# Two heads' score products in the row halves of TensorE, and first weights split ahead of the first group's rows: attention and two expert layers on one core

## The reference

```python
scores = scale * np.matmul(q, k.transpose(0, 1, 3, 2))
kth = np.partition(scores, -top_k, axis=-1)[..., -top_k:-top_k + 1]
mask = scores >= kth
scores = np.where(mask, scores, -1000000000.0)
scores = scores - np.max(scores, axis=-1, keepdims=True)
attn = np.exp(scores)
attn = attn / (np.sum(attn, axis=-1, keepdims=True) + 1e-09)
...
for e in range(E):
    mask = e_idx == e
    h = np.maximum(x[mask] @ w1[e], 0.0)
    out[mask] = gate_w[mask, None] * (h @ w2[e])
...
for e in range(E):
    h = np.maximum(x @ w1[e], 0.0)
    out += p[:, e:e + 1] * (h @ w2[e])
```

## Time and profile before

| | |
|---|---|
| median of 3 runs | 956.07 us (955.36 to 958.46) |
| the profiled execution | 953.17 us, its span 951.4 us |
| TensorE busy | 903.7 us, 95% of the span |
| VectorE busy | 557.8 us, 59% |
| ScalarE busy | 340.6 us, 36% |
| GpSimd busy | 286.1 us, 30% |
| mean granted TensorE clock | 0.957 of 2.4 GHz |

### The profile page before, as it was taken

One profiled execution on the slowest core, in us unless ns is written; L12 is line 12 of the kernel. 1 busy time (PEld: TensorE's weight loads), 2 busy tenths in 40 slices (PEclk: granted clock), 3 DMA queues, 4 the chain that ended last, 5 costly groups with the idle time before them and its releaser, 6 DMA issues.

```text
span 951.4 us, 13448 instructions
## 1 busy us (share of the span) xinstructions
PE 903.7 (95%) x4813; PEld 758.7 (80%) x4813; DVE 557.8 (59%) x1103; ACT 340.6 (36%) x726; POOL 286.1 (30%) x231
## 2 busy tenths in 40 slices
PE   5999999997999999993899799999999999999998
PEld 4888888886767667662778699989998998889897
DVE  4999999999999989752365334233223321332121
ACT  3545555553546555413364411212112220222010
POOL 7676667646775665304111020000000000000000
PEclk8589999996999999987999999999999999999999
DMA  9130000005332434325548160022002100000001
GB/s 221 48 111 23 7 18 12 12 13 198 123 111 100 163 113 147 118 95 186 191 145 288 36 243 1 1 89 89 1 1 89 54 34 0 0 0 0 33 11 55
DMA packets 49395, 75.61 MB, mean 79 GB/s; under 512 B 24624, under 2 KB 24624, under 8 KB 49328
## 3 DMA queue, kind: packets, MB, share of 16 engines
q1 hardware_dynamic: 42160, 61.09, 18.7%
q0 software_dynamic: 4160, 13.63, 4.6%
q10 hardware_dynamic: 3008, 0.05, 0.2%
HBM read 63.49 MB, written 11.27 MB: 79 GB/s over the span
## 4 chain that ended last, share of the span: by engine, by line
PE 75%; issue 10%; POOL 9%; DMA 3%; SPq 1%; DVE 1%; ACT 1%; PEld 1%; PEldq 0%; POOLq 0%; DVEq 0%; ACTq 0%
PE bank L1376 19%; PE bank L1377 18%; PE bank L1378 18%; PE bank L1432 6%; POOL att L633 6%; PE bank L1511 4%; PE bank L1371 4%; PE bank L1527 3%; POOL att L636 2%; PE bank L1403 2%; PE bank L1401 1%; DMA w_raw<-in_moe_w_dram 1%; DMA q_raw<-in_q_dram 1%; DMA xs_raw<-x_a,a_tok_i 1%; PE bank L1540 1%
## 5 line engine op out<-in xcount | busy, mean ns | idle before, releaser
L633 POOL TENSOR_SCALAR att<-sc,top 128x576 f32<-128x576 f32 x70 | 120.8, 1726 | 122.2 <-DVE top L1060 111.4
L1060 DVE MAX8 top<-work 128x8 f32<-128x576 f32 x216 | 152.0, 743 | 0.1
L1376 PE MATMUL bank<-xT,w1h 128*128 128x384 f32 x384 | 129.3, 337 | 5.3 <-DVE w1l L1255 5.3
L1313 DVE SCALAR_TENSOR_TENSOR hT<-bank,hT 128x384 fp32r<-128x384 f32 x96 | 52.9, 557 | 130.5 <-ACT hT L957 130.1
L1378 PE MATMUL bank<-xT,w1h 128*128 128x384 f32 x384 | 128.9, 336 | 0.0
L1377 PE MATMUL bank<-xT,w1l 128*128 128x384 f32 x384 | 128.9, 336 | 0.0
L957 ACT ACTIVATE hT<-bank 128x384 fp32r<-128x384 f32 x96 | 46.9, 492 | 200.5 <-PE bank L1378 200.5
L1376 PE MATMUL bank<-w2h,hT 128*128 128x512 f32 x288 | 112.2, 390 | 1.2 <-DVE hT L1313 1.2
L1432 PE MATMUL bank<-v_one,attT 128*128 128x65 f32 (+3 forms) x800 | 111.7, 281 | 0.8 <-ACT av L768 0.6
L1378 PE MATMUL bank<-w2l,hT 128*128 128x512 f32 x288 | 112.2, 390 | 0.0
L1377 PE MATMUL bank<-w2h,hT 128*128 128x512 f32 x288 | 112.2, 389 | 0.0
(11 more groups left out here) (266 smaller groups left out, 1524.0 us busy)
## 6 DMA issues: line engine op xcount, KB each, us to landing
w_raw<-in_moe_w_dram SPq DMA_DIRECT2D x96, 512.0 KB, 6.0
q_raw<-in_q_dram SPq DMA_DIRECT2D x18, 128.0 KB, 2.7
v_one<-in_v_dram POOLq DMA_DIRECT2D x18, 128.0 KB, 5.8
out_dram<-x_tok SPq DMA_DIRECT2D x9, 256.0 KB, 2.0
k_raw<-in_k_dram SPq DMA_DIRECT2D x8, 256.0 KB, 5.2
y_dram<-zero POOLq DMA_DIRECT2D x2, 1024.0 KB, 6.7
y_dram<-b_ys POOLq DMA_DIRECT2D x7, 256.0 KB, 2.8
x_dram<-x_cur SPq DMA_DIRECT2D x6, 256.0 KB, 7.1
```

Of the source, the lines that this page charges most:

```text
L633: nc.gpsimd.tensor_scalar(att[:, g % ATR, :], sc[:, g % RING, :], top8[:, g % RING, 3, 7:8], None, ALU.is_ge).then_inc(keep_made, 1)
L1060: nxt = nc.vector.max(out=top8[:, g % RING, i + 1, :], in_=work[:, j, :])
L1313: nc.vector.scalar_tensor_tensor(out=hTl(b)[:, f, :], in0=bank[:, HB + f % 4, 0:BW], scalar=0.0, in1=f32(hTh(b)[:, f, :]), op0=ALU.max, op ...
L1376: nc.tensor.matmul(dst, high_lhs, high_rhs, start=start, stop=False)
```

## The change

1. `scores(p)` makes, at an even step p, the first 288 columns of the two heads p and p + 1, and at the odd step the other 288 columns of both. The six matmuls of a step alternate between the partition halves, one head's product into bank `SB`, the other's into `SB + 1`. The count of matmuls and their shapes stay.
2. `copy_scores` writes half the columns of two buffers instead of one whole buffer; at an even step it waits until one more head is done before it overwrites. VectorE now starts both heads of a pair when the second step's copy is made.
3. In tile 4 `att_times_v` alternates between the two column halves of the array for each chunk of the contraction, instead of finishing one half first.
4. `dense_products` gives 5 instead of 4 outside tile 4, 3 instead of 2 where only the scores are of tile 4, 4 instead of 2 where only the values' product is, and 2 instead of 0 where both are.
5. Where attention ends ScalarE splits the first piece of weights, then makes the exponentials, then splits the other three, and only then copies group a's fifth result.

```diff
+        def pair_half(p):
+            return p - p % 2, slice(p % 2 * HS, (p % 2 + 1) * HS)
...
-            def copy_scores(g):
-                act.wait_ge(sc_made, g + 1)
-                if g >= RING:
-                    act.wait_ge(att_made, g - RING + 1)
-                nc.scalar.activation(sc[:, g % RING, :].rearrange("p (a b) -> p a b", a=2), bank[:, SB:SB + 2, 0:HS],
+            def copy_scores(p):
+                g, cols = pair_half(p)
+                act.wait_ge(sc_made, p + 1)
+                if p == g and g >= RING:
+                    act.wait_ge(att_made, g + 1 - RING + 1)
+                nc.scalar.activation(sc[:, g % RING:g % RING + 2, cols], bank[:, SB:SB + 2, 0:HS],
...
-            act.wait_ge(GB.lsub_made, 3)
-            nc.scalar.activation(GB.lg_b[:, :, :], GB.lg_a[:, :, :], ACT.Exp).then_inc(GB.lexp_made, 1)
             with act.If(guarded(act, GA, SPREAD)):
+                group_exponents()
+                a_copy_y(SPREAD - 1)
                 a_rare_slots()
+                split_high(0, w1_raw, w1h, w1_loaded, w1_high)
             with act.Else():
+                split_high(0, w1_raw, w1h, w1_loaded, w1_high, (0,))
+                group_exponents()
+                split_high(0, w1_raw, w1h, w1_loaded, w1_high, (1, 2, 3))
+                a_copy_y(SPREAD - 1)
                 act.drain().then_inc(a_ys, GA.slots - SPREAD)
-            split_high(0, w1_raw, w1h, w1_loaded, w1_high)
...
-                    dve.wait_ge(sc_copied, g + 1)
+                    dve.wait_ge(sc_copied, g0 + 2)
...
-                for i in range(2):
-                    cols = slice(i * HS, (i + 1) * HS)
-                    for j, (high, low, b) in enumerate(parts):
-                        last = product(bank[:, SB + i, 0:HS], high[pp, h // 2, :], low[pp, h // 2, :],
-                                       kTh[b][pp, h // 2, cols], kTl[b][pp, h // 2, cols], j == 0, j == len(parts) - 1)
+                pairs = [both for high, low, b in parts for both in ((high, kTh[b]), (low, kTh[b]), (high, kTl[b]))]
+                for j, (query, key) in enumerate(pairs):
+                    for i in range(2):
+                        pp = slice(D * i, D * i + D)
+                        last = nc.tensor.matmul(bank[:, SB + i, 0:HS], query[pp, c, :], key[pp, c, cols], start=(j == 0), stop=(j == len(pairs) - 1))
...
-                for r0, r1, b in rows:
-                    for c in range(KC):
-                        kk = P if c < KC - 1 else KL
+                for c in range(KC):
+                    kk = P if c < KC - 1 else KL
+                    for r0, r1, b in rows:
...
-                return 4 - 2 * (p // H == SPLIT) - 2 * ((p - AV_LAG) // H == SPLIT)
+                return 5 - 2 * (p // H == SPLIT) - ((p - AV_LAG) // H == SPLIT)
```

More of the change, by code:

```diff
@@ L831, in beside @@
                         a_copy_xT(s + 1)
-                yield from clock.until(A_START + A_STEP * SPREAD)
-                a_copy_y(SPREAD - 1)
             def a_rare_slots():
@@ L897, in _, with group_exponents @@
                 pass
-            act.wait_ge(GB.lsub_made, 3)
-            nc.scalar.activation(GB.lg_b[:, :, :], GB.lg_a[:, :, :], ACT.Exp).then_inc(GB.lexp_made, 1)
+            def group_exponents():
+                act.wait_ge(GB.lsub_made, 3)
+                nc.scalar.activation(GB.lg_b[:, :, :], GB.lg_a[:, :, :], ACT.Exp).then_inc(GB.lexp_made, 1)
             with act.If(guarded(act, GA, SPREAD)):
+                group_exponents()
+                a_copy_y(SPREAD - 1)
                 a_rare_slots()
+                split_high(0, w1_raw, w1h, w1_loaded, w1_high)
             with act.Else():
+                split_high(0, w1_raw, w1h, w1_loaded, w1_high, (0,))
+                group_exponents()
+                split_high(0, w1_raw, w1h, w1_loaded, w1_high, (1, 2, 3))
+                a_copy_y(SPREAD - 1)
                 act.drain().then_inc(a_ys, GA.slots - SPREAD)
-            split_high(0, w1_raw, w1h, w1_loaded, w1_high)
             def xT_high_part(t):
@@ L1404, in transpose_att, with scores @@
                 last.then_inc(attT_made, 1)
-            def scores(g):
-                t, h = g // H, g % H
-                pp = slice(D * (h % 2), D * (h % 2) + D)
+            def scores(p):
+                g, cols = pair_half(p)
+                t, c = g // H, g % H // 2
                 parts = [(qTh[:, t % 2], qTl[:, t % 2], 0 if t <= SPLIT else 1)]
@@ L1411, in scores @@
                     parts.append((mixed_h, mixed_l, 1))
-                if h == 0:
+                if p % H == 0:
                     pe.wait_ge(turn_read, turn_use["ql", t])
-                if g >= 1:
-                    pe.wait_ge(sc_copied, g)
-                for i in range(2):
-                    cols = slice(i * HS, (i + 1) * HS)
-                    for j, (high, low, b) in enumerate(parts):
-                        last = product(bank[:, SB + i, 0:HS], high[pp, h // 2, :], low[pp, h // 2, :],
-                                       kTh[b][pp, h // 2, cols], kTl[b][pp, h // 2, cols], j == 0, j == len(parts) - 1)
+                if p >= 1:
+                    pe.wait_ge(sc_copied, p)
+                pairs = [both for high, low, b in parts for both in ((high, kTh[b]), (low, kTh[b]), (high, kTl[b]))]
[3 more added lines that the diff above has]
+                        last = nc.tensor.matmul(bank[:, SB + i, 0:HS], query[pp, c, :], key[pp, c, cols], start=(j == 0), stop=(j == len(pairs) - 1))
                 last.then_inc(sc_made, 1)
```

## The result

The changed kernel takes 931.72 us (median of 4 runs, 929.68 to 932.31), the kernel before in the same series 957.27 (4 runs, 955.36 to 961.72): a ratio of 0.9723, 95% interval 0.9684 to 0.9762. The forecast was 931.5 us. The profiled execution took 931.97 us with a span of 930.0, which was 951.4 before: 21.4 us less where 24.6 were forecast.

A forecast was written before the change was run, and what follows sets the result against it. TensorE and VectorE both full early (VectorE counts), TensorE in the dense stage, a chain of waits where attention ends. 0.6 + 0 + 14.6 + 9.4 = 24.6 us less: 928.6 profiled, 931.5 in the runs, range 926 to 948.

The forecast's parts named there:

- Scores, 0.39 us a step: Score matmuls: both row halves run at once, three of six starts go, saving 3 x 0.13 = 0.39 us a step.
- The three rivals to it: Scores: weights one after another, 947 (0.16); no overlap, 956.7 (0.08); changing halves costs like changing shape, 984 (0.10).
- Filling: Steps 8 to 34: extra products cost 11.6 us, scores give back 12.5; this stretch neither gains nor loses.
- TensorE's lead: First stretch, head 35: TensorE is 1.55 us ahead of VectorE; slowed by more, it sets the pace.
- Start: First pair of heads: faster scores give 1.4 us, VectorE's new wait costs 0.76; net 0.6 us less.
- Two steps of faster scores at half the clock give about 2 x 0.7 = 1.4: At the start: the first two score steps, at half the clock, save about 1.4 us.
- Dense stage: Steps 43 to 71, TensorE dense: scores 11.3 and tile 4's values 3.3, together 14.6 us saved.
- 29 x 0.39 = 11.3: Steps 43 to 71: 29 score steps saving 0.39 us each, 11.3 us.
- 3 x 1.1 = 3.3: Tile 4's product with the values, steps 43 to 45: alternating column halves saves 1.1 us each, 3.3 us.
- VectorE's cap of 15.1 us: From 245 to 405: VectorE waits 15.1 us for TensorE, so it follows a faster one by that at most.
- Where attention ends: ScalarE's new order lets the gather start 10.4 us earlier; less 1.0 for stalls, 9.4 us saved.
- about two such stalls in 4.7 us make the indices 1.0 later (0 to 2): Where attention ends: GpSimd's work beside VectorE's small operations delays the indices 1.0 us, bounds 0 to 2.

The follow-up runs named there:

- the run without packing: Changed kernel with score products, their copies and VectorE's wait as before; new filling, tile 4 order and end kept: 955.82 us, ratio 0.9986.
- the one with the old filling count: Changed kernel with the kernel before's number of filling products (4, not 5, outside tile 4): 931.57 us, ratio 0.9735.
- the run with the late store: Changed kernel, but SyncE stores group a's fifth result only after asking for the second weights: 929.09 us, ratio 0.9707.
- both mended: Changed kernel with VectorE making all four low pieces of the first weights and SyncE storing the fifth result after requesting the second weights: 926.24 us, ratio 0.9676.

## Why the forecast held, and where it was off

**Scores, 0.39 us a step: right,** the one figure that no row had shown. It was measured as such in the early step, and the kernel without it gains nothing. The three rivals to it fall: loads don't come one after another but together, and no score matmul follows the one before after 0.22 us. What I had not thought of is that the overlap didn't need the order to alternate. On what was forecast from the Trainium skill, "TensorEngine Tiling (Array Packing)", Key Properties (changing the mode drains, changing the tile doesn't): the trace agrees, 0.01 us between halves, and 0.22 us still from scores to values (105.18 - 104.96).

**Filling: right.** The copy that completes the scores of heads 34 and 35 starts at 186.03 instead of 187.59, 1.6 us sooner (0.9 forecast), VectorE doesn't wait between 60 and 190, and the first mark is at 229.23 against 229.07. Alone the product costs 11.0 us up to that mark (10.1 forecast, TensorE's lead taken off).

**Start: 0.6 forecast, nothing measured.** The step that failed is "Two steps of faster scores at half the clock give about 2 x 0.7 = 1.4". ScalarE and VectorE in the changed kernel, then TensorE and ScalarE before:

```profile
17.93 0.65 ACT L750 ACTIVATE sc<-bank 128x576 f32<-128x576 f32 x1 [3.49 <-PE bank L1433]
19.76 0.65 ACT L750 ACTIVATE sc<-bank 128x576 f32<-128x576 f32 x1 [1.18 <-PE bank L1433]
20.44 1.42 DVE L1058 MAX8 top<-sc 128x8 f32<-128x576 f32 x2 [3.74 <-ACT sc L750]
```

```profile
16.46 0.37 PE L1376 MATMUL bank<-kTh,qTh 64*128 64x288 f32 x1 [2.48 <-DVE kTl L1006]
...
17.85 0.65 ACT L745 ACTIVATE sc<-bank 128x576 f32<-128x576 f32 x1 [3.24 <-PE bank L1378]
```

From copy to copy it is 1.83 us instead of 2.55: the second step gave its 0.72, the first nothing. The wait takes just that back: both MAX8 are done at 21.86, before at 21.84. The first step gave nothing for two reasons. In the trace of before its first matmul took 0.37 us, the length at the full clock, where the next step's took 0.61, so from it to the copy it was 1.39 us, and 1.13 after: 0.26 won and not 0.7. And in the changed kernel's execution the step began 0.34 us later, at 16.80, behind an earlier operation of VectorE. In two runs in which both steps are slow and begin at 16.48 and 16.53, the first copy starts at 18.29 without overlap and at 17.65 with it (the run without packing and the one with the old filling count). So the 1.4 us are there at equal clocks; I had priced both steps at half the clock without looking at the first one's row.

**Dense stage: 14.6 forecast, 14.7 measured, but one part by luck.** 29 x 0.39 = 11.3 for the scores stands. For tile 4's values 3 x 1.1 = 3.3 was worked out from 2.85 us, a row at half the clock, which I took for the rule. By the rows it is (2.85 + 1.80 + 1.80) - (1.52 + 0.95 + 0.95) = 3.0 here, of which 0.5 are there because one product met the half clock in both traces. The halves overlap almost fully (0.85 of 0.9 us), not by four fifths as I had assumed. The clock has a part in the 14.7 as well. The changed kernel's stage holds 3.4 us at half the clock, by its 0.66 from 230 to 235, and the run with the late store, which has none, takes 1.2 us less (170.4). The kernel before holds 6.3 us, up to 235.4. In proportion that is 2.2 us, so about 1.0 of the 14.7 is the clock's and 13.7 the change's, beside 11.3 + 3 x 0.85 = 13.9 from the rows. That is an estimate from single executions. VectorE's cap of 15.1 us was close: its waits for score copies are gone.

**Where attention ends: 9.4 forecast, 6.6 measured.** The order worked as forecast, the sizes didn't. The main step that failed is "about two such stalls in 4.7 us make the indices 1.0 later (0 to 2)". They were two, but each waits for the end of a whole subtraction, 1.67 us instead of 0.31 and 1.87 instead of 0.17 (in the kernel before; with all low pieces on VectorE 0.31 and 0.18), and the indices came 2.8 later, outside my bound. The pair of the earlier trace rows that the bound was taken from doesn't show the same operation twice: one writes 24 columns, the other 8. Then 0.5 because the gather follows the first of the indices by 1.0 us instead of 0.5. And 0.6 because from the gather to the request for the weights it is 6.3 us instead of 5.8: SyncE waits for `ys` first, whose product fell into a stretch of half clock (5.38 us for eight instead of 3.68), a wait that before had been over by then. At the full clock it would have been 5.2 with the store first (the run with the old filling count) and 4.9 with the store behind, as the gather's own issue is 1.0 us shorter than before (1.05, before 2.02). 9.4 - 1.8 - 0.5 - 0.6 = 6.5. I had moved ScalarE's copy back and looked at who waits for its buffer, but not at who stands behind its store.

The Trainium skill, "SBUF — State Buffer", Who interferes with whom, says that VectorE and GpSimd share one pair of ports as an exclusive lock: an operation of VectorE that works in a two-port mode, or that has two inputs in SBUF while GpSimd's reads SBUF too, and the one of GpSimd exclude each other for the whole instruction. The trace agrees: 1.67 and 1.87 us, both ending with the subtraction. By that rule the bound of such a stall is GpSimd's own 2.3 us and not the 0.65 of the earlier trace rows.

**The total.** 0 + 0 + 14.7 + 6.6 = 21.3 of span, 24.6 forecast. That the median came out at 931.72 beside 931.5 is in part luck: the span fell by 3.2 us less than forecast, and the medians of the series lie 25.5 us apart, some 4 more than the two spans, which about makes up for it.

## What to carry to other kernels

Matmuls that use half the rows or half the columns of the array should come from both halves in turns (for row halves a few places of the queue were near enough): each pair then costs about what one did (0.60 us instead of 0.99 for a step of six). Before a row's length goes into a sum, its granted clock is to be read beside it, and the row taken where the clock is that of the stretch it is used for. Work of GpSimd that is moved beside VectorE's small steps can cost the rest of a whole GpSimd instruction for each step that it blocks (1.67 and 1.87 us here), and where a copy is moved, its store and what stands behind it in the queue have to be followed too. With both mended the kernel took 926.24 us beside 931.72, in different series.

## What the runs showed of the hardware

- TensorE starts a matmul of the idle row half ahead of older ones that wait for the busy half: three places ahead in steps of six (303.98), and in tile 4 once three of six were gone (174.80). With ten records of one column half ahead of the other's nothing overlapped (1.80 us).
- In turns, column halves overlap like row halves, with fp32 operands and their loads: 20 records in 0.95 us instead of 1.80.
- A cast of 18 columns took 1.87 us beside GpSimd's subtraction, and 0.17 to 0.18 without it; the reduction between the two stalled operations took 0.30 either way.
- The same instructions ran at either clock in different executions. With ScalarE's old order the clock was 0.50 from 395 to 410, and the dense stage was 4.5 us longer; group a's last product took 5.38 or 3.68 us, and the request for the second weights moved by 1.1. Differences of that size between single spans were read by stage, not as a whole.
